# Attention and MLP on one core: all products with the first matrix ahead of those with the second, and a home for all rows of the relu tiles

## The reference

```python
# attention, per batch (4) and head (8), 576 rows, head width 64
scores = scale * q @ k.T
scores = where(scores >= max(scores) - tau, scores, -1e9)   # per row
x = softmax(scores) @ v                                     # heads side by side: 576 x 512
# MLP, per batch
u  = x + (x.T @ U @ V).T
ch = maximum(u @ w_ch1, 0.0) @ w_ch2                        # 512 -> 2048 -> 512
z  = u + ch
# then a third stage sends each row of z to one of 8 experts
```

## Time and profile before

| | us |
|---|---|
| median of 3 runs (lowest to highest) | 1206.09 (1204.56 to 1208.46) |
| the profiled execution, its own time | 1202.22 |
| its span | 1199.7 |
| TensorE busy in the span | 1084.5 (90%) |
| VectorE, ScalarE, GpSimd busy | 587.6, 438.0, 345.5 |
| mean granted TensorE clock | 0.968 of full |

### The profile page before, as it was taken

How to read it: one execution, slowest core, us unless ns; L and a number is a source line. 1 busy time by engine, 2 the same in 40 slices (tenths; PEclk the granted TensorE clock), 3 DMA queues, 4 the chain that set the end, 5 groups by cost and what they waited for, 6 DMA issues and landing times. The chain is left out here.

```text
span 1199.7 us, 20063 instructions
## 1 busy us (share of the span) xinstructions
PE 1084.5 (90%) x7110; PEld 948.3 (79%) x7111; DVE 587.6 (49%) x1155; ACT 438.0 (37%) x719; POOL 345.5 (29%) x322
## 2 busy tenths in 40 slices
PE   3677789999999999998999989899947999999996
PEld 2555579989978989997998989699946788788785
DVE  1366555575545655655566653222248335254641
ACT  1355453333344434335433322311143334244531
POOL 2355103254330533541054424044211112112111
PEclk9999999999999999998999989899966999999998
DMA  6666503252442424336052311122056345153611
GB/s 147 148 164 161 121 1 89 86 155 63 119 134 62 120 73 127 109 92 168 17 148 62 101 54 44 66 72 71 1 198 205 135 159 184 45 174 121 207 65 37
DMA packets 111449, 129.16 MB, mean 108 GB/s; under 512 B 67373, under 2 KB 67373, under 8 KB 111344
## 3 DMA queue, kind: packets, MB, share of 16 engines
q1 hardware_dynamic: 106160, 116.15, 34.3%
q0 software_dynamic: 3520, 10.75, 2.8%
q10 hardware_dynamic: 1664, 0.89, 0.3%
HBM read 87.90 MB, written 10.22 MB: 82 GB/s over the span
## 5 line engine op out<-in xcount | busy, mean ns | idle before, releaser
L757 ACT ACTIVATE ex<-score_banks,stat 128x576 f32<-128x576 f32 x131 | 97.0, 740 | 206.8 <-DVE stat L855 206.8
L651 PE MATMUL mlp_banks<-u_hi,w_hi 128*128 128x320 f32 (+1 forms) x512 | 158.1, 309 | 7.6 <-DVE hid_lo L914 4.7
L659 PE MATMUL mlp_banks<-hid_hi,w_hi 128*128 128x320 f32 (+1 forms) x512 | 157.6, 308 | 7.7 <-DVE z L922 7.2
L482 POOL TENSOR_TENSOR w_lo<-stage,w_hi 128x1024 fp32r<-128x1024 f32 x64 | 152.7, 2386 | 4.6
L651 PE MATMUL mlp_banks<-u_hi,w_lo 128*128 128x320 f32 (+1 forms) x512 | 152.2, 297 | 0.0
L651 PE MATMUL mlp_banks<-u_lo,w_hi 128*128 128x320 f32 (+1 forms) x512 | 152.1, 297 | 0.0
L659 PE MATMUL mlp_banks<-hid_hi,w_lo 128*128 128x320 f32 (+1 forms) x512 | 151.4, 296 | 0.0
L659 PE MATMUL mlp_banks<-hid_lo,w_hi 128*128 128x320 f32 (+1 forms) x512 | 151.3, 295 | 0.0
L478 POOL CAST w_hi<-stage 128x1024 fp32r<-128x1024 f32 x64 | 66.5, 1038 | 269.9 <-PE mlp_banks L651 231.9
L865 DVE SCALAR_TENSOR_TENSOR ex<-score_banks,stat,ex 128x576 f32<-128x576 f32 x131 | 106.9, 816 | 60.6 <-ACT ex L757 49.6
L586 PE MATMUL score_banks<-k_tiles,q_tiles 128*128 128x288 f32 x580 | 106.3, 311 | 28.5 <-ACT et_first L767 12.3
(11 more groups left out here) (230 smaller groups left out, 2012.5 us busy)
## 6 DMA issues: line engine op xcount, KB each, us to landing
stage<-in_moe_w_ch SPq DMA_DIRECT2D x64, 512.0 KB, 3.9
w_raw<-in_moe_w SPq DMA_DIRECT2D x64, 512.0 KB, 5.3
q_tiles<-q_parts SPq DMA_DIRECT2D x32, 320.0 KB, 3.9
q_tiles<-q_parts SPq DMA_DIRECT2D x64, 160.0 KB, 4.2
k_tiles<-k_parts SPq DMA_DIRECT2D x60, 144.0 KB, 3.5
raw_q<-in_q SPq DMA_DIRECT2D x32, 128.0 KB, 2.4
raw_v<-in_v SPq DMA_DIRECT2D x32, 128.0 KB, 2.7
raw_k<-in_k SPq DMA_DIRECT2D x30, 128.0 KB, 2.8
```

Of the source, the lines that this page charges most:

```text
L482: nc.gpsimd.tensor_tensor(w_lo[:, n % RING], stage[:, n % 2], w_hi[:, n % RING].bitcast(F32), ALU.subtract).then_inc(w_split, 1)
L651: last = nc.tensor.matmul(bank[:, 0:w], ch1(a, g, d, c), of[:, d, cols], start=(d == 0 and n == 0), stop=(d == KC - 1 and n == 2))
L659: last = nc.tensor.matmul(bank[:, 0:w], ch2(a, g, q, c), of[:, q, 0:w], start=(q == 0 and n == 0), stop=(q == QUARTER - 1 and n == 2))
L757: nc.scalar.activation(ex_of(n), score_of(n), ACT.Exp, bias=stat[:, n % 4, 0:1], scale=-1.0).then_inc(exp_done, 1)
```

## The change

The list of a group is written with all eight hidden tasks first (k = 0, then k = 1) and then all eight channel tasks. `hid_hi` and `hid_lo` get a column for each of the 576 rows in place of 320, so that both halves can lie in them at once, and all that reads or writes them is shifted by the start of the half. The last reader of a piece of the first matrix is now task 7 of a group in place of task 11, and `last_user` says so. Waits of TensorE for emptied tiles are counted anew.

```diff
@@ mlp_tasks
     for r in range(NQ):
         for k in range(2):
             tasks += [("hidden", k, r, q) for q in range(QUARTER)]
+        for k in range(2):
             tasks += [("channel", k, r, c) for c in range(KC)]
@@ last_user
-    return b * NTASK + GROUP0 + r * PER_GROUP + (PER_GROUP // 2 + QUARTER - 1 if i < 2 else PER_GROUP - 1)
+    return b * NTASK + GROUP0 + r * PER_GROUP + (2 * QUARTER - 1 if i < 2 else PER_GROUP - 1)
@@ attention_and_mlp
-    hid_hi = sb("hid_hi", [P, QUARTER, WMAX], F32R)
-    hid_lo = sb("hid_lo", [P, QUARTER, WMAX], F32R)
+    hid_hi = sb("hid_hi", [P, QUARTER, S], F32R)
+    hid_lo = sb("hid_lo", [P, QUARTER, S], F32R)
@@ TensorE, channel
                     if c == 0:
-                        pe.wait_ge(dve_task, emptied(BY_DVE, t - QUARTER + q))
+                        pe.wait_ge(dve_task, emptied(BY_DVE, t - 2 * QUARTER + q))
...
-                        last = nc.tensor.matmul(bank[:, 0:w], ch2(a, g, q, c), of[:, q, 0:w], start=(q == 0 and n == 0), stop=(q == QUARTER - 1 and n == 2))
+                        last = nc.tensor.matmul(bank[:, 0:w], ch2(a, g, q, c), of[:, q, START[k]:START[k] + w], start=(q == 0 and n == 0), stop=(q == QUARTER - 1 and n == 2))
@@ TensorE, logits
-                pe.wait_ge(dve_task, emptied(BY_DVE, b * NTASK + NTASK - TAIL - 1 - (1 - k) * (QUARTER + KC)))
+                pe.wait_ge(dve_task, emptied(BY_DVE, b * NTASK + NTASK - TAIL - 1 - (1 - k) * KC))
@@ ScalarE, hidden
-                nc.scalar.activation(hid_hi[:, c, 0:w], bank[:, 0:w], ACT.Relu).then_inc(act_task, 1)
+                nc.scalar.activation(hid_hi[:, c, START[k]:START[k] + w], bank[:, 0:w], ACT.Relu).then_inc(act_task, 1)
@@ VectorE, hidden
-                nc.vector.scalar_tensor_tensor(out=hid_lo[:, c, 0:w], in0=bank[:, 0:w], scalar=0.0, in1=hid_hi[:, c, 0:w].bitcast(F32),
+                nc.vector.scalar_tensor_tensor(out=hid_lo[:, c, START[k]:START[k] + w], in0=bank[:, 0:w], scalar=0.0, in1=hid_hi[:, c, START[k]:START[k] + w].bitcast(F32),
```

## The result

The changed kernel is slower: 1225.74 us in the median of four runs (1224.69 to 1227.86) against 1205.32 for the kernel before in the same comparison (1203.44 to 1208.46). The ratio is 1.0172, its 95% interval 1.0151 to 1.0193. The forecast was 1226.7, its range 1207 to 1241. The profiled execution took 1225.93, against 1202.22.

The account below looks back on a forecast made before the run. TensorE, near nine tenths busy, bounds the kernel; GpSimd bursts holding small VectorE operations cause its few stalls. Stalls +14.6 and clock falls +6 give 1222.8 us profiled, plus 3.9 makes 1226.7 median; range 1207 to 1241.

Parts of the forecast that it names:

- What bounds it: TensorE is busy 50.00 us of 50 in the MLP alone, so the new task order itself can win little.
- (a): Steps 55, 91, 127 (j = 1): bursts move one step earlier, removing three waits of 2.41 us, a gain of 7.2 us.
- (b): Bursts of steps 48, 84, 120 move to 46, 82, 118 (j = 1): stalls of 3.05 us, three times, 9.2 us.
- (c): Steps 64, 100, 136 (j = 1): loads come in time, stalls 2.95, 2.95 and 3.63, 9.5 us against 4.7 before.
- (d): Steps 50, 86, 122 (j = 5): earlier loads make bursts hold the tau addition, stalls of 1.3 us, three times.
- (e): Bursts of steps 70, 106, 142 move to 68, 104, 140 (j = 5): stalls of 1.3 us, three times.
- (f): Bursts moving from step 63 to 61 and its like, 57 and 72: one held tau addition at most, costing nothing.
- The clock: Behind five new stalls of about 3 us: half bring falls to 1.2 GHz at 2.4 us each, 6 us; bounds 0 to 12.
- The sum: Whole kernel: stalls +14.6 and clock +6 give +20.6 us, 1222.8 profiled, plus 3.9 makes a median of 1226.7.
- The first: Rival: VectorE's tau addition slips ahead of GpSimd's first subtraction; all slip: 1191.8 us, chance 0.09; only six: 1206 to 1209, 0.06.
- The second: Rival: at j = 5 the inverse loses to GpSimd's second subtraction in six steps; 1241 to 1255 us, chance 0.10.
- The third: Rival: loads still come late or GpSimd's release is later, so only (a) and (b) happen; 1212 us, chance 0.07.

Follow-up runs that it names:

- kernel 1: The changed kernel with the old, later release of the first matrix's pieces (task 11 of a group), keeping the new order and wide tiles: 1205.98 us, ratio 1.0005.
- kernel 2: The kernel before, with SyncE issuing the load of a weight piece one step earlier: 1224.83 us, ratio 1.0163.
- Kernels 5: The changed kernel, with GpSimd's burst released one task later where the step after has j = 1 or 5: 1191.74 us, ratio 0.9874.
- kernel 7: The changed kernel, with tau added to the row minimum as a scalar operand instead of a second tensor: 1189.44 us, ratio 0.9863.
- Kernel 6: The kernel before, with GpSimd's burst released one task later where the step after has j = 1 or 5: 1187.43 us, ratio 0.9854.
- kernel 3: The changed kernel without the addition of 1e-9, so the reciprocal reads the row sums directly: 1202.09 us, ratio 0.9962.

## Why the prediction was right

**What bounds it, and that the order wins nothing.** This was right: kernel 1 shows 1.0005, and the MLP alone kept its 50.00 of 50; from its first hidden matmul to its last channel matmul it took 102.6 us, for 103.1 before.

**The stalls, step by step.** **(a)** was right: there is no wait at 55, 91, 127, which wins 7.2 us. **(b)** gave 3 x 2.96 = 8.9 us for the forecast 9.2. **(c)** gave 2.98, 2.97 and 3.62 for 2.95, 2.95 and 3.63, and kernel 2 shows by itself that it is enough for the loads to come in time. **(d)** and **(e)** gave 1.13 to 1.15 each for 1.3. In (d) TensorE goes on 221.87 - 215.89 = 5.98 us after the step's start, for 6.0 forecast; it only arrived 0.16 later than I took it to. I had the inverse wait for the second cast and slip in behind it. It ran its usual 0.17 us, beginning under the cast (to 220.68) and ending just behind it. **(f)** cost nothing, as said. The stalls after are 25.3 us for 26.5.

**The clock.** The sum came out nearly right from two wrong sizes, which is luck. The step said that half of five falls come, at 2.4 each, 6 in all. All five came, at 1.3 to 1.6 each, 7.5, and the one at 136 went from 2.4 to 1.6 as well, so 6.7 net. That 3 us lies midway between 2.41 and 3.63 was no reason for a half: in the traces of before, of the change and of kernels 1 and 2 each of the eleven stalls of 2.96 us or more brought the clock down, and of the nine of 2.41 one did. That a fall costs 2.4 was taken for the rule from one case, step 136 in before, which cost 0.8 more than any of the others behind stalls.

**The sum.** +14.6 and +6 were forecast; +13.4 and +6.7 were found. The profiled execution came out at 1225.93, for 1222.8; the longer experts' stage is more than the whole difference. The median came out at 1225.74, for 1226.7. I had carried over the 3.9 us by which the runs of before lay above their profile, and after the change the profile lies at the median. So that the median was met within 1 us is in part luck: 3.9 us too much and an experts' stage that I had not counted nearly cancel.

**The rivals.** The first was that VectorE slips in ahead of the first subtraction. It did not at any of the twelve steps: it came 0.10 to 0.12 us too late at the steps released by a channel task, as before (217.31 against 217.41), and 0.44 at the others. Kernels 5 and 7 reach what it would have given (1191.8 forecast; 1191.74, 1189.44), so its price was right. The second was that the inverse at j = 5 loses to the second subtraction. It did not: the twelve 4-column inverses of the changed kernel ran 167 ns in the mean. It was decided by 0.03 us, so that the chance of 0.10 was not too high. The third was that the loads come late. They did not: GpSimd has no wait for the MLP's DMA.

**The shared port pair.** The Trainium skill (SBUF — State Buffer, section "SBUF: two separate sides", on the shared port pair) says that VectorE contends in a two-port mode or with two SBUF inputs, and that the other engine then waits for the whole instruction. The tau line fits: with two SBUF inputs it is held up to 2324 ns, and with tau as a scalar it takes 217 at most. The inverse has one SBUF input and is held too; by that sentence it would be in a two-port mode, which no run here shows. The prediction left open who goes first when VectorE waits and GpSimd has its next instruction ready. Kernel 6 shows it again, as the earlier trace rows did: an inverse that started under the cast ended at 243.39, and the subtraction began at 243.45, behind it.

## What to carry to other kernels

Releasing a buffer earlier is not a gain by itself. It sets when another engine starts, and if that engine can hold a small operation which stands ahead of others in a queue, the early start costs the whole chain behind it. So look in the trace for tiny operations whose longest duration is many times their median, see which instruction of another engine ends with them, and first change their form (here a second tensor operand to a scalar), then the moment of the other engine's work. And a late load in the profile may be what keeps two engines apart: before it is hurried, ask what it will then collide with.

## What the runs showed of the hardware

- The addition of tau as a tensor-scalar operation of 128x1 was never held by GpSimd (108 of 108 at 205 to 217 ns in kernel 7, 45 of them begun beside a subtraction). The tensor-scalar addition of 1e-9 was held, for up to 2.29 us at 128x6 and up to 0.80 at 128x4, and so was the tensor-tensor addition of 128x1, for up to 2.32. The reciprocal of 128x6, all in SBUF, was not held (191 ns in the mean of 12 in kernel 3). So the number of SBUF inputs alone does not decide. The two tensor-scalar additions differ in their columns and in their scalar (a column of tau, a constant), and no run takes these apart.
- A held operation of VectorE gets in between two instructions of GpSimd that follow each other at once, and costs GpSimd nothing that shows: between the cast and the subtraction lie 0.08 us with an operation held (243.37 to 243.45 in kernel 6) and without (191.88 to 191.96 in the changed kernel).
- Stalls of TensorE of 2.96 to 2.98 us brought the clock to 1.2 GHz seven times of seven (five in the changed kernel, two in kernel 2), those of 2.41 us once in nine times. A fall cost 1.3 to 1.6 us behind either (5.05 for 3.48 us behind step 64; in kernel 2 460.99 - 455.27 = 5.72 behind step 91, for 253.78 - 249.64 = 4.14 behind step 55), and once, in before at step 136, 2.4.
